# A recurrent attention and two expert layers: first layer in pairs of steps, two blocks' normalisation moved to the second

## What is computed

```python
def _moe_ref(x, w_in, w_out, a, b):          # w_in 320 x 2048
    h = x @ w_in
    h2 = h * h
    h3 = h2 * h
    P = a[0] + a[1] * h + a[2] * h2 + a[3] * h3
    Q = 1.0 + np.abs(b[0]) * np.abs(h) + np.abs(b[1]) * h2
    return (P / (Q + 1e-06)) @ w_out
def _moe2_ref(x, w_gate, w_val, w_out, rms_g):   # 320 x 1536
    rms = np.sqrt(np.mean(x * x, axis=-1, keepdims=True) + 1e-06)
    xn = x / rms * rms_g
    g = xn @ w_gate
    silu = g * (1.0 / (1.0 + np.exp(-g)))
    return (silu * (xn @ w_val)) @ w_out
```

## Time and profile before

| | us |
|---|---|
| time before, median of 3 runs (lowest to highest) | 555.93 (554.12 to 560.58) |
| the profiled execution's own time | 559.43 |
| its span | 557.6 |
| attention, to the first matmul of the first layer | 138.7 |
| first layer's last `second` ends | 350.6 |

### The profile page before, as it was taken

How to read it: one execution, slowest core, us unless ns; L and a number is a source line. 1 busy time by engine, 2 the same in 40 slices (tenths; PEclk the granted TensorE clock), 3 DMA queues, 4 the chain that set the end, 5 groups by cost and what they waited for, 6 DMA issues and landing times.

```text
span 557.6 us, 7929 instructions
## 1 busy us (share of the span) xinstructions
PE 496.4 (89%) x2582; PEld 430.0 (77%) x2582; DVE 349.1 (63%) x630; ACT 308.2 (55%) x595; POOL 251.8 (45%) x268
## 2 busy tenths in 40 slices
PE   1599799789699999899997899589999999999996
PEld 1388678688489888678876798478888888888886
DVE  6256786377689999689987796544344333343343
ACT  3946664352699998889986996524322121212121
POOL 6045764232488888988889776624410000000000
PEclk9998985778899999999999899789999999999999
DMA  6545764323000000000110101122201000010001
GB/s 216 139 126 158 208 190 143 93 73 93 0 12 17 21 14 13 12 13 12 42 30 0 29 1 29 33 69 69 58 2 37 11 1 1 0 48 1 1 0 48
DMA packets 29409, 28.76 MB, mean 52 GB/s; under 512 B 14424, under 2 KB 23000, under 8 KB 29368
## 3 DMA queue, kind: packets, MB, share of 16 engines
q1 hardware_dynamic: 29368, 28.26, 17.3%
HBM read 26.28 MB, written 1.97 MB: 51 GB/s over the span
## 4 chain that ended last, share of the span: by engine, by line
PE 50%; POOL 18%; DVE 9%; issue 8%; DMA 8%; ACT 4%; SPq 2%; POOLq 0%; DVEq 0%; ACTq 0%
PE ps L1085 6%; PE ps L1087 6%; PE ps L1086 6%; DMA q_pair<-q_p_dram 6%; POOL qq L437 6%; POOL g_lo L444 5%; PE ps L1053 4%; PE ps L1055 4%; PE ps L1054 4%; PE ps L963 4%; PE ps L990 3%; PE ps L1089 3%; PE ps L1090 3%; DMA sig_o<-o_n_dram 2%; DVE qr L838 2%
## 5 line engine op out<-in xcount | busy, mean ns | idle before, releaser
L1053 PE MATMUL ps<-wo_hi,g_hi 128*128 128x320 f32 x336 | 105.5, 314 | 9.2 <-POOL g_lo L444 6.5
L1055 PE MATMUL ps<-wo_hi,g_lo 128*128 128x320 f32 x336 | 104.5, 311 | 0.0
L1054 PE MATMUL ps<-wo_lo,g_hi 128*128 128x320 f32 x336 | 104.4, 311 | 0.0
L676 ACT ACTIVATE cc<-ps 128x512 f32<-128x512 f32 x36 | 21.5, 598 | 136.8 <-PE ps L1090 136.8
L896 DVE TENSOR_TENSOR pp<-ps,cc 128x512 f32<-128x512 f32 x36 | 24.9, 691 | 91.4 <-ACT cc L676 91.4
L437 POOL TENSOR_TENSOR qq<-qq,ab 128x512 f32<-128x512 f32 x48 | 62.1, 1294 | 33.3 <-ACT qq L604 30.1
L1053 PEld LDWEIGHTS ps<-wo_hi,g_hi 128*128 128x128 f32 x336 | 63.6, 189 | 14.7 <-issue 8.8
L1054 PEld LDWEIGHTS ps<-wo_lo,g_hi 128*128 128x128 f32 x336 | 63.7, 190 | 2.8
L444 POOL TENSOR_TENSOR g_lo<-g,g_hi 128x512 fp32r<-128x512 f32 x48 | 62.1, 1295 | 4.4 <-ACT g_hi L624 3.9
L1055 PEld LDWEIGHTS ps<-wo_hi,g_lo 128*128 128x128 f32 x336 | 63.7, 190 | 0.0
L1085 PE MATMUL ps<-x_hi,w2b_hi 128*128 128x512 f32 x132 | 52.9, 401 | 6.6 <-POOLq L411 6.6
(11 more groups left out here) (150 smaller groups left out, 1135.5 us busy)
## 6 DMA issues: line engine op xcount, KB each, us to landing
stage<-w_in_dram SPq DMA_DIRECT2D x20, 384.0 KB, 3.1
stage<-w_out_dram SPq DMA_DIRECT2D x8, 320.0 KB, 4.4
k_pair<-k_p_dram SPq DMA_DIRECT2D x12, 208.0 KB
q_pair<-q_p_dram SPq DMA_DIRECT2D x12, 208.0 KB
kn<-k_n_dram SPq DMA_DIRECT2D x12, 208.0 KB, 3.7
q_diag<-q_t_dram SPq DMA_DIRECT2D x24, 80.0 KB
v<-v_n_dram SPq DMA_DIRECT2D x12, 160.0 KB, 4.3
sig_o<-o_n_dram SPq DMA_DIRECT2D x2, 960.0 KB, 9.7
```

What stands on the lines that cost most here:

```text
L1053: pe.matmul(acc[t], hi, hi_w[:, f, :], start=(f == 0), stop=False)
L1054: pe.matmul(acc[t], hi, lo_w[:, f, :], start=False, stop=False)
L1055: mm = pe.matmul(acc[t], lo, hi_w[:, f, :], start=False, stop=(f == FT - 1))
```

## The change

The first layer goes in 24 pairs of steps. `slope`, `log_q`, `inverse`, `high` on ACT and `newton_1`, `newton_2`, `quotient` on DVE take a pair at once, 1024 columns; `absolute`, `linear`, the numerators, and POOL's `denominator` and `low` stay at 512 columns, two each. The first quotient fills two PSUM banks (6 and 7), so nothing can be transposed beside it; blocks 1 and 2 keep their raw rows (`raw`, over x_lo) and are squared, multiplied, scaled, transposed and split in the second layer (squares in its step 1, transposes at steps 6, 8, 18 and 20, `TURNS`). Block 0's squares and gains stay in the first layer (pairs 12 to 16), its transposes come at the layer's end. PE takes `second` six steps behind `first` (LAG1 = 6). Only four in2 pieces are split in the first layer (by POOL, pairs 1 to 4); the other eight in2 pieces and all twelve out2 pieces are split in the second layer, in turns, out2 f and in2 f + 4, ACT rounding up to two pieces a step. With two staging buffers and this order the in2 pieces come through one and the out2 pieces through the other until in2 is done.

```diff
 NU = 2 * NT
-SQUARES = 4
-TURN = 9
-LAG1, LAG2 = 4, 2
+LAG1, LAG2 = 6, 2
+EARLY = 4
+NP = NB * FT1 // 2
+PB = FT1 // 2
+TURNS = (6, 8, 18, 20)
...
+        x_lo = at("x_lo", [P, NB, KT, TB], F32R)
+        raw = at("raw", [P, NB, KT * TB], F32, offset=x_lo_at)
...
+        qq = [at(f"qq{i}", [P, 2, TB]) for i in range(2)]
+        low_at = []
+        cc = []
+        for i in range(4):
+            low_at.append(cursor[0])
+            cc.append(at(f"cc{i}", [P, 2, TB]))
+        g_lo = [at(f"g_lo{i}", [P, 2, TB], F32R, offset=low_at[i]) for i in range(4)]
+        g_hi = [at(f"g_hi{i}", [P, 2, TB], F32R) for i in range(3)]
         xs = at("xs", [P, TT, KT * P])
...
+        FA = (229344 - cursor[0]) // tile2
+        w2_a = w2_tiles("w2a", FA)
...
+        FB = (wo1_at - cursor[0]) // tile2
+        w2_b = w2_tiles("w2b", FB)
+        cursor[0] = wo1_at
+        w2_c = w2_tiles("w2c", FT2 - FA - FB)
+
...
         hp = [ps[:, 4, :], ps[:, 5, :]]
-        r0 = ps[:, 6, :]
+        r0 = ps[:, 6:8, :]
...
+        def second_set(n):
+
+            return (n + sum(1 for p in TURNS if p < n)) % 2
...
+            if t < TT:
+                return ps[:, 4 + t % 2, 0:KT * P].rearrange("p (k l) -> p k l", l=P)
+            p = TURNS[(t - TT) // 2]
+            other = (second_set(p) + 1) % 2
+            return ps[:, 4 + 2 * other + t % 2, 0:KT * P].rearrange("p (k l) -> p k l", l=P)
...
-        pieces += [("in2", f, 1) for f in range(FT2)]
+        pieces += [("in2", f, 1) for f in range(EARLY)]
+        for f in range(FT2):
+            pieces.append(("out2", f, 1))
+            if EARLY + f < FT2:
+                pieces.append(("in2", EARLY + f, 1))
         piece_of = {}
...
+            def denominator(m):
+
+                pool.wait_ge(z_done, m + 1)
+                for h in range(2):
+                    pool.tensor_tensor(qq[m % 2][:, h, :], qq[m % 2][:, h, :], ab[m % 2][:, h, :], ALU.mult)\
+                        .then_inc(q_done, 1)
+
+            def low(m):
+
+                pool.wait_ge(ghi_done, m + 1)
+                for n in (2 * m, 2 * m + 1):
+                    pool.tensor_tensor(glo(n), cc[m % 4][:, n % 2, :], ghi(n).bitcast(F32), ALU.subtract)\
+                        .then_inc(glo_done, 1)
...
+            def gains(t):
+
+                pool.wait_ge(acc_read, t + 1)
+                if t >= TT:
...
+                pool.tensor_tensor(xs[:, t % TT, HD:], raw_part(t)[:, 2 * P:], gain[:, 2 * P:], ALU.mult)
+                pool.tensor_tensor(xs[:, t % TT, 0:HD], raw_part(t), gain[:, :], ALU.mult).then_inc(gained, 1)
...
-                if n % 3 == 2 and piece < first_w2b:
+            for k in range(NP + 2):
+                if k < NP:
+                    denominator(k)
+                if k >= 2:
+                    low(k - 2)
+                if PB + 4 <= k < PB + 4 + TT:
+                    gains(k - PB - 4)
+                if k == PB + 4 + TT:
+                    rms(slice(0, TT), 1)
+                if 1 <= k <= EARLY:
                     split(piece)
                     piece += 1
             pool.wait_ge(glo_done, NB * FT1)
-            split(piece)
-            for t in range(TT):
-                gains(NB - 1, t)
-            rms(NB - 1)
-            for n in range(piece + 1, len(pieces)):
+            for n in range(4):
+                split(LATE + n)
+            rms(slice(TT, NT), 2)
+            for t in range(TT, 2 * TT):
+                gains(t)
+            for n in range(LATE + 4, len(pieces)):
                 split(n)
+            for t in range(2 * TT, NT):
+                gains(t)
...
-
-                act.wait_ge(act_h, 2 * n + 1)
-                if n >= 2:
...
+            def slope(m):
+
...
-
-            def inverse(n):
-
...
+            def log_q(m):
+                act.wait_ge(q_done, 2 * m + 2)
+                act.activation(ab[m % 2][:, :, :], qq[m % 2][:, :, :], ACT.Ln, bias=one_eps[:, 0:1])\
+                    .then_inc(ln_done, 1)
...
+            def inverse(m):
...
+                act.wait_ge(ln_done, m + 1)
+                if m >= 1:
...
+                act.activation(r0, ab[m % 2][:, :, :], ACT.Exp, scale=-1.0).then_inc(r0_done, 1)
...
+            def high(m):
+                act.wait_ge(g_done, m + 1)
+                if m >= 3:
+                    act.wait_ge(out_done, 2 * m - 4)
+                act.activation(g_hi[m % 3][:, :, :], cc[m % 4][:, :, :], ACT.Copy).then_inc(ghi_done, 1)
...
+            def squares(t):
+                act.wait_ge(acc_read, t + 1)
...
+            for k in range(NP + 2):
+                if k < NP:
+                    absolute(2 * k)
+                    linear(2 * k)
+                if 1 <= k <= NP:
+                    log_q(k - 1)
+                    inverse(k - 1)
+                if k >= 2:
+                    high(k - 2)
+                if k < NP:
+                    absolute(2 * k + 1)
+                    linear(2 * k + 1)
+                    slope(k)
+                if k in (PB + 4, PB + 5):
                     for t in range(2):
-                        squares(j - 1, 2 * (f - SQUARES) + t)
-                if 0 < j < NB and f == SQUARES + TT // 2:
-                    rms_start(j - 1)
-                if 0 < j < NB and turned(f) is not None:
-                    hi_of_x2((j - 1) * TT + turned(f))
-
-
-            act.wait_ge(out_done, (NB - 1) * FT1 + W2B_OVER)
-            round_piece(first_w2b)
-            high(NB * FT1 - 1)
+                        squares(2 * (k - PB - 4) + t)
+                if k == PB + 6:
+                    rms_start(slice(0, TT), TT)
+                if k == NP:
+                    hi_of_x2(0)
+                    hi_of_x2(1)
+            hi_of_x2(2)
+            hi_of_x2(3)
+            round_piece(LATE)
...
+            piece = LATE + 1
             for n in range(NB * FT2 + 1):
                 if n < NB * FT2:
                     sigmoid(n)
                 if n >= 1:
                     high2(n - 1)
-                if first_w2b + 1 + n < len(pieces):
-                    round_piece(first_w2b + 1 + n)
+                for _ in range(2):
+                    if piece < len(pieces):
+                        round_piece(piece)
+                        piece += 1
                 if n == 1:
-                    for t in range(TT):
-                        squares(NB - 1, t)
+                    for t in range(TT, NT):
+                        squares(t)
                     act.preload_act_table_set("natural_log_exp_and_others")
-                    rms_start(NB - 1)
-                if n == 2:
-                    for t in range((NB - 1) * TT, NB * TT):
-                        hi_of_x2(t)
+                    rms_start(slice(TT, NT), NT)
+                if n in TURNS:
+                    t = TT + 2 * TURNS.index(n)
+                    hi_of_x2(t)
+                    hi_of_x2(t + 1)
...
-                                         ALU.add, ALU.mult).then_inc(ch_done, 1)
+                part = cc[n // 2 % 4][:, n % 2, :]
+                dve.scalar_tensor_tensor(part, part, coef_a[:, 2:3], hp[n % 2], ALU.add, ALU.mult).then_inc(ch_done, 1)
...
-                dve.scalar_tensor_tensor(qr[:, :], qq[n % 2][:, :], one_eps[:, 0:1], r0, ALU.add, ALU.mult)\
-                    .then_inc(qr_done, 1)
...
-            def newton_2(n):
-                dve.wait_ge(qr_done, n + 1)
-                dve.scalar_tensor_tensor(r0, qr[:, :], 2.0, r0, ALU.subtract, ALU.mult).then_inc(nr_done, 1)
...
-            def quotient(n):
-                dve.wait_ge(nr_done, n + 1)
-                if n >= 3:
...
-                dve.scalar_tensor_tensor(g[n % 3][:, :], pp[n % 2][:, :], coef_a[:, 0:1], r0,
+                part = cc[n // 2 % 4][:, n % 2, :]
+                dve.scalar_tensor_tensor(part, part, coef_a[:, 1:2], hp[n % 2], ALU.add, ALU.mult).then_inc(p_h, 1)
...
+            def newton_1(m):
+
...
+                                         ALU.add, ALU.mult).then_inc(qr_done, 1)
...
+                dve.wait_ge(gained, t // TT * TT + TT)
+                dve.tensor_tensor(x_part(x_lo, t), turn_bank(t), x_part(x_hi, t).bitcast(F32), ALU.subtract)\
                     .then_inc(xlo_done, 1)
...
+            for k in range(NP + 1):
+                if k < NP:
+                    numerator_1(2 * k)
+                    numerator_2(2 * k)
+                if k >= 1:
+                    newton_1(k - 1)
+                if k < NP:
+                    numerator_1(2 * k + 1)
+                    numerator_2(2 * k + 1)
+                if k in (PB + LAG1 // 2 - 1, 2 * PB + LAG1 // 2 - 1):
+                    read_acc(k // PB - 1)
+                if k >= 1:
+                    newton_2(k - 1)
+                    quotient(k - 1)
+                if PB + 5 + TT <= k < PB + 7 + TT:
+                    for t in range(2):
+                        scale_rows(2 * (k - PB - 5 - TT) + t)
+            for t in range(TT):
+                lo_of_x2(t)
...
```

(99 more changed lines are left out.)

349 lines of the change are left out of this document (140 added, 209 removed).

## The result

The changed kernel took 620.73 us (median of 4 runs, 617.71 to 624.61) against 558.25 for the kernel before in the same session: a ratio of 1.115, 95% interval 1.104 to 1.126. Forecast were 638 us and a range of 600 to 662. One kernel's executions differ by 1 to 3%, at a lower or higher granted clock; all ratios and intervals here compare the faster executions of both kernels, while the profiles of before, early6, halves and halves_spread are of slower ones.

A forecast was written before the change was run, and what follows sets the result against it. A loop through PE, ACT and POOL bounds the first layer: 167.0 start, 21 pairs at 11.65, an end of 15 to 17, to 427.7; plus 212 for the second layer, 639.7 of span, 638 us on the median; range 600 to 662.

The forecast's parts named there:

- Part 2, the chain: First layer: PE's first, ACT's slope, POOL's two denominators and low, then PE's second form one loop, 10.13 us a pair.
- Part 4, the start: First layer before its steady pairs: second(0) put at 167.0, where it was 156.7 before.
- Part 3, the clock: PE's clock around its 2.9 us pauses: 10.13 us a pair always full, 13.2 always half, middle 11.65 taken.
- the same chain, the clock stays full: Rival, first layer: the loop through g_lo at full PE clock, 605 us of span, 603 us on the median's scale; chance 0.18.
- the upper bound: First layer with PE's clock always half, lengthening first and second in the loop: 13.2 us a pair.
- Part 5, the second layer: Second layer: net +5 us, 212 in all, with bounds 0 and +15.
- first stall: Second layer: second2(1) waits behind ACT's eight squares and table loads, about 3 us, 6.6 before.
- the supply: Second layer: all eight in2 pieces go through one of two staging buffers, some 8 us by step 10.
- The cover of the early splits: First layer, pairs 1 to 4: in2 splits bring POOL to 9.6 us, hidden under 10.1; otherwise they cost 4 x 2.4 us.
- The 8.1 loop: Rival, first layer: ACT and POOL alone close a loop from slope to slope, 8.1 us a pair, 562 us; chance 0.05.

The follow-up runs named there:

- early6: Changed kernel with six in2 pieces instead of four split by POOL in the first layer: 623.72 us, ratio 1.112 to the kernel before.
- halves: Changed kernel with slope in two 512-column operations and POOL alternating one denominator and one low: 584.07 us.
- halves_spread: Changed kernel with slope halved, POOL alternating, newton_2 and quotient ahead of numerators, early in2 splits one operation a pair: 562.56 us, ratio 0.9986 to the kernel before.
- run 1: Changed kernel with POOL taking low ahead of the two denominators: 584.74 us, ratio 1.055 to the kernel before.
- run 2: Changed kernel with LAG1 = 7 instead of 6, so PE wants each g_lo one step later: 581.04 us, ratio 1.048 to the kernel before.
- Run 3: Changed kernel with one more 64-column POOL product between denominators and low in 22 pairs: 641.29 us, ratio 1.157 to the kernel before.
- pause_more: Same as Run 3: changed kernel with one more 64-column POOL product ahead of low in 22 pairs, 641.29 us.
- squares_spread: Changed kernel with the second layer's squares four each in steps 1 and 2, table loads in step 3, POOL's gains later: 616.82 us, ratio 1.111 to the kernel before.
- low_first: Same as run 1: changed kernel with POOL taking low ahead of the denominators, 584.74 us.
- run 5: Changed kernel with LAG1 = 7 and DVE taking newton_2 and quotient ahead of the odd step's numerators: 566.49 us, ratio 1.014 to the kernel before.

## Why the prediction was right, and where its size was off

**Part 2, the chain: right, to 0.05 us.** Forecast 10.13 a pair; the timeline above has it as 262.49 - 252.32 = 10.17. `first` to its result took 2.02 (254.15 to 256.17), ACT 2.34 (256.17 to 258.51), POOL with its start 3.83 (258.51 to 262.34), the handover 0.15, and `second` 1.83 (252.32 to 254.15) where 1.76 was put. Runs 1 and 2 cut it at its two ends and both freed it. (The POOL term of the sum is 0.08 + 3 x 1.27 = 3.89, not 3.87.) The size of the 1024-column operations came out too: slope 1.24, log_q 1.15, inverse 1.03, high 1.04 against 1.24, 1.15, 1.02, 1.05.

**Part 4, the start: right, in part by luck.** `second(0)` at 166.6, forecast 167.0; but the layer had begun 1.4 earlier than was assumed, so its start took 1.0 longer than worked out. From `second(42)` (388.86) to the end of `second(47)` (407.2) it took 18.3, forecast 16.

**Part 3, the clock: the term that was mis-sized.** "No row decides; I take the middle, 11.65." Measured were 10.58 on average: 21 x 1.07 = 22.5 us too much; 22.5 + 0.4 at the start - 2.3 at the end = 20.6 is the whole difference in the first layer (427.7 forecast, 407.2 measured). Seventeen of 21 pairs ran at full clock. The rival "the same chain, the clock stays full" (603 us) was as near as my forecast: the result lies between them, and that it fell into the range owes something to how wide this open term had made it. Run 3 shows how little would have changed the answer: with 0.25 us more rest the average is 11.77. What the Trainium skill says in "TensorE: Matmul & The Clock Gate", that throttling is the default and activity releases it, I had read as speaking for the upper bound. Here activity kept the clock in most pairs: the changed kernel lies 0.45 us a pair above its full-clock chain (10.58 - 10.13) and pause_more 1.39 above its own (11.77 - 10.38), of the 3.1 that half clock throughout would have cost (13.2 - 10.13).

**Part 5, the second layer: the sum right by luck.** Forecast +5, measured +4.5. I had a first stall of about 3 us (3.4 measured), set off against the 6.6 of before, and put some 8 us on the supply through one staging buffer. Such a loss in waits is not there: PE's listed waits in this layer are 6.8 us against 8.2 before (6.6 and 1.6), and its busy time is 5.7 us longer, with 1.4 worked out for the transposes. ACT did wait for transfers (15.5 us for in2 pieces from 407 on), but PE stood still for only 3.2 us ahead of `first2(7)`, and early6, with fewer pieces to come, left that wait as it was. squares_spread took the burst from ACT, moved POOL's order with it, and gained 4.9 us, most of it in the clock. So the supply was argued and was wrong as the main term; how the 5.7 divide into clock and work, no run here separates.

**The cover of the early splits.** "Were the chain gone, they would cost 4 x 2.4 us": in low_first the first pairs took 9.77, as said (167.18 to 176.95); the gain of spreading them was only 3.5 us of 9.6.

**The 8.1 loop: a rival in its own right.** Given 5% as the outcome, its size was what runs 1, 2 and 5 found under the chain (8.35, 8.11, 8.02). Its path binds in run 5 alone: in run 1 it was the loop through `low`, in run 2 the one through newton_2, by 0.1.

## What to carry to other kernels

A lag counted in steps says nothing; follow one value around all the in-order lists and add up the time from an instruction to the next one of its kind that must wait for it, then divide by how many steps lie between. Merging two steps into one operation makes each list shorter and each such loop longer, so after a merge every list needs its order worked out again: here `low` before `denominator`, and the odd step's numerators between the Newton step and the quotient. When no engine is busy over 80% and all wait for each other about once a period, look for the loop before looking at any operation's size; and when one loop is cut, work out the next, because four lay within 1 us of each other here (8.34, 8.11, 8.02 and, on average, 7.5).
